# Attention stage of an attention and mixture-of-experts kernel: x kept in SBUF and stored late, k and v products by 128 tokens, two score buffers, normalization on GpSimd

## What is computed

```python
# attention over a memory of 32 slots, for 8 batches x 8 heads, 576 tokens, 64 dims
a = exp(phi - max(phi, tokens)); a = a / (sum(a, tokens) + 1e-9)       # [b h s m]
k_m, v_m = einsum('bhsm,bhsd->bhmd', a, k), einsum('bhsm,bhsd->bhmd', a, v)
scores = q @ k_m.T / sqrt(64); scores -= max(scores, m)
attn = exp(scores); attn = attn / (sum(attn, m) + 1e-9)
x = (attn @ v_m)                       # heads joined: x is [4608 tokens, 512]
# feed-forward, 512 -> 2048 -> 512
h = x @ w_in; x2 = (h * sigmoid(1.702 * h)) @ w_out
# 8 experts, 512 -> 1024 -> 512, each token by the one of its largest logit
e = argmax(x2 @ w_gate); gate = softmax(x2 @ w_gate)[e] * sigmoid(x2 @ w_output_gate)[e]
out = gate * (relu(x2 @ w1[e]) @ w2[e])
```

## Time and profile before

| | |
|---|---|
| device time, median of 3 runs | 1362.95 us (1360.7 to 1366.06) |
| the profiled execution: its own time | 1360.2 us |
| its span, first to last instruction | 1358.1 us |
| mean granted TensorE clock | 0.998 |
| TensorE busy | 1321.8 us, 97% |
| VectorE, ScalarE, GpSimd busy | 660.8, 388.8, 527.6 us |
| HBM read, written | 146.03 MB, 100.45 MB |

### The profile page before, as it was taken

The page is one execution under the profiler, slowest core; times in us unless marked ns, Lnnn a source line. Parts: engine busy times, 40 slices in busy tenths (PEclk is TensorE's granted clock), DMA queues, the critical chain, the costliest instruction groups (busy, mean ns, idle before and its releaser), DMA issues.

```text
span 1358.1 us, 25712 instructions
## 1 busy us (share of the span) xinstructions
PE 1321.8 (97%) x7778; PEld 1075.4 (79%) x7779; DVE 660.8 (49%) x1349; ACT 388.8 (29%) x721; POOL 527.6 (39%) x622
## 2 busy tenths in 40 slices
PE   6888999999999999999999999999999999999997
PEld 4566788888888888888888888887788888888886
DVE  5997243453433433434334344347655555555553
ACT  3554222232222222322223222223322222222221
POOL 2005774453344433433434435511433342433331
PEclk9999999999999999999999999999999999999999
DMA  8996447656565465454654646547873779649882
GB/s 322 391 409 251 139 153 206 201 193 184 189 193 182 160 192 188 169 186 155 185 193 159 184 175 192 176 148 258 238 226 96 219 227 266 169 125 250 259 238 62
DMA packets 155641, 275.28 MB, mean 203 GB/s; under 512 B 17107, under 2 KB 54244, under 8 KB 153540
## 3 DMA queue, kind: packets, MB, share of 16 engines
q1 hardware_dynamic: 98804, 205.35, 44.0%
q10 hardware_dynamic: 43600, 37.37, 11.2%
q0 software_dynamic: 13184, 31.88, 7.5%
HBM read 146.03 MB, written 100.45 MB: 181 GB/s over the span
## 4 chain that ended last, share of the span: by engine, by line
PE 93%; DMA 2%; POOL 1%; ACT 1%; issue 1%; DVE 0%; ACTq 0%; SPq 0%; POOLq 0%; DVEq 0%
PE ps L674 28%; PE ps L707 28%; PE ps L748 16%; PE ps L777 15%; PE ps L633 2%; PE ps L620 1%; PE ps L648 1%; PE ps L717 1%; DMA x2x<-xT_scratch 1%; DMA raw<-in_moe_w_out 1%; PE ps L605 1%; DMA kvm<-in_kv 1%; DMA xT_scratch<-xo 1%; POOL W L1509 0%; POOL xs L1538 0%
## 5 line engine op out<-in xcount | busy, mean ns | idle before, releaser
L674 PE MATMUL ps<-xs,W 128*128 (+1 forms) x1728 | 417.8, 391 | 3.1 <-POOL W L1519 1.6
L707 PE MATMUL ps<-W,gs 128*128 128x512 f32 x1728 | 415.0, 389 | 0.1
L674 PEld LDWEIGHTS ps<-xs,W 128*128 128x128 f32 x1728 | 322.8, 188 | 73.0 <-issue 4.4
L707 PEld LDWEIGHTS ps<-W,gs 128*128 128x128 f32 x1728 | 324.2, 188 | 67.9 <-DVE gs L1205 0.5
L1203 DVE TENSOR_TENSOR gate<-ps,gate 128x512 f32<-128x512 f32 x144 | 99.6, 691 | 358.8 <-ACT gate L931 358.4
L931 ACT ACTIVATE gate<-ps 128x512 f32<-128x512 f32 x144 | 86.1, 598 | 466.3 <-PE ps L674 465.8
L748 PE MATMUL ps<-W,cx 128*128 (+1 forms) x936 | 218.5, 389 | 0.8 <-issue 0.8
L777 PE MATMUL ps<-W,chT 128*128 (+1 forms) x936 | 218.3, 389 | 0.9 <-DVE chT L1340 0.9
L1546 POOL CAST whi<-raw 128x512 fp32r<-128x512 f32 x128 | 85.4, 667 | 319.0 <-DMA raw<-in_moe_w 318.9
L777 PEld LDWEIGHTS ps<-W,chT 128*128 128x128 f32 x936 | 175.5, 188 | 38.1 <-issue 1.7
L748 PEld LDWEIGHTS ps<-W,cx 128*128 128x128 f32 x936 | 175.5, 188 | 37.6 <-issue 1.4
(11 more groups left out here) (158 smaller groups left out, 810.4 us busy)
## 6 DMA issues: line engine op xcount, KB each, us to landing
W<-expert_scratch SPq DMA_DIRECT2D x24, 2048.0 KB, 11.0
raw<-in_moe_w SPq DMA_DIRECT2D x128, 256.0 KB, 2.8
expert_scratch<-whi SPq DMA_DIRECT2D x128, 256.0 KB, 2.6
expert_scratch<-raw SPq DMA_DIRECT2D x128, 256.0 KB, 2.9
cq<-ch ACTq DMA_DIRECT2D x156, 128.0 KB, 3.8
kvm<-in_kv SPq DMA_DIRECT2D x16, 1152.0 KB, 7.1
crec<-record_scratch POOLq DMA_DIRECT2D x160, 64.0 KB, 3.7
qT<-in_q SPq DMA_DIRECT2D x16, 576.0 KB, 6.3
```

What stands on the lines that cost most here:

```text
L674: mm = pe.matmul(ps[:, f % 2, :], W[:, col:col + P], xs[:, bass.ds(x0 + (x_lo * K1 + c) * T, T)], start=(c == 0 and w_lo + x_lo == 0), sto ...
L707: mm = pe.matmul(ps[:, 2 + s, :], gs[:, f % 2, g_lo, s * P:(s + 1) * P], W[:, col:col + DM], start=(f == 0 and g_lo + w_lo == 0), stop=(f ...
```

## The change

- **x kept.** `x_out` copies the attention output of batches 0 to 6 into a buffer `keep` that lies where w_out's half of W comes to lie, and of batch 7 into `xo`. Nothing of x is stored during the groups. ScalarE stores batches 0 to 5 in two DMAs within group 15, batch 6 in two more behind it (`store_kept`), batch 7 in one (`store_last`). GpSimd's split of the first chunk into the `keep` region beyond the first four (f == 4) waits for the stores; SyncE's `load_x(1)` waits for the first of them.
- **Tile 0 of x** is split out of `keep` and isn't loaded: high parts by ScalarE (`first_x_hi`, in group 15), low parts by GpSimd (`first_x_lo`, three) and VectorE (one).
- **k and v products by 128 tokens.** CA = 4 chunks of 128 tokens, and 64 tokens left over: 16 + 4 products instead of 36, four 128x128 transposes and two small ones instead of 18. The host lays out kv and phi to match, in rows of the same length.
- **Next a transposed early.** `exp_phi(g+1)` and the transposes of a for g+1 move into group g, ahead of the k transpose and the scores of g.
- **Two score buffers** `sc[u]`. VectorE's order becomes `phi_in(g+1)`, `inverses(g)` (sums and inverses for the scores of g-2 and, in one more column, for phi of g), `less_max(g-1)`, `attn_out(g-2)`.
- **GpSimd** does the normalizing multiply (`normalize(g-2)`, after `inverses(g)`) and the v blocks (`v_blocks(g)`, from SBUF, scaled by `kv_scale(g)` on ScalarE, which scales k and v in one instruction).
- **Layout of w_in** and of the x rows by 128-row blocks instead of every fourth row; early weight chunks are loaded behind groups 1, 2, 11 and 12.

```diff
-CA = 9
-PA = S // CA
+CA = S // P
+PA = S - CA * P
...
+        KEEP = SLOT // 2
+        KEPT = B - 1
...
-                if not isinstance(g, int) or g >= 4:
-                    store_group(g, b, u)
...
-                if isinstance(g, int) and g < K1 - 1:
-                    load_w(g, w_in_part(g, 0))
-                if isinstance(g, int) and g == NG - 5:
-                    load_w(K1 - 1, w_in_part(K1 - 1, 0))
+                if isinstance(g, int) and 1 <= g < 3:
+                    load_w(g - 1, w_in_part(g - 1, 0))
+                if isinstance(g, int) and g >= NG - 5 and g < NG - 3:
+                    load_w(g - (NG - 5) + 2, w_in_part(g - (NG - 5) + 2, 0))
...
                         if k == 1:
+                            sp.wait_ge(s_xfirst, 16 * 2)
+                            sp.wait_ge(s_pT, NG)
                             load_x(t + 1)
...
+            def a_transposes(g):
+                wait(pe, s_aT, g + 1)
+                for c in range(CA):
+                    pe.transpose(ps[:, 0, c * P:(c + 1) * P], aT[:, c * P:(c + 1) * P], ident[:])
+                for hh in range(2):
+                    rows = slice(hh * PA, (hh + 1) * PA)
+                    tr = pe.matmul(ps[rows, 1, 0:PA], aT[rows, CA * P:S], ident[rows, rows],
+                                   start=True, stop=True, tile_position=(hh * PA, hh * PA))
+                tr.then_inc(s_atr, 1)
             def group(g, b, r):
                 u = r % 2
                 has_out = not isinstance(g, int) or g >= 2
-                wait(pe, s_aT, g + 1)
+                last = isinstance(g, int) and g == NG - 1
+                wait(pe, s_kvl[u], 16 * (b + 1))
+                if not isinstance(g, int) or g >= 3:
+                    wait(pe, s_xo, 2 * g - 5)
+                hold(pe, s_am, g + 1)
+                out_of = lambda h: ps[h * M:(h + 1) * M, 4, 3 * P:4 * P].rearrange("p (w d) -> p w d", w=2)
+                for c in range(CA):
+                    for h in range(HG):
+                        pe.matmul(out_of(h), am[:, c * P + h * M:c * P + (h + 1) * M], kv_main[u][:, :, h, c, :],
+                                  start=(c == 0), stop=False, tile_position=(0, h * M))
+                for h in range(HG):
+                    hh, h2 = h // 2, h % 2
+                    rows = slice(hh * PA, (hh + 1) * PA)
+                    mm = pe.matmul(out_of(h), am[rows, CA * P + h2 * M:CA * P + (h2 + 1) * M], kv_left[u][rows, :, h2, :],
+                                   start=False, stop=True, tile_position=(hh * PA, h * M))
+                mm.then_inc(s_kv, 1)
+                if not last:
+                    a_transposes(g + 1)
                 wait(pe, s_kmT, g)
-                hold(pe, s_vbd, g)
-                for c in range(CA):
-                    for hh in range(2):
-                        rows = slice(hh * PA, (hh + 1) * PA)
-                        tr = pe.matmul(ps[rows, c // 8, (c % 8) * 2 * M:(c % 8 + 1) * 2 * M], aT[rows, c * PA:(c + 1) * PA],
-                                       ident[rows, rows], start=True, stop=True, tile_position=(hh * PA, hh * PA))
-                tr.then_inc(s_atr, 1)
+                hold(pe, s_kk, g + 1)
+                for i in range(2):
+                    tr = pe.matmul(ps[i * D:(i + 1) * D, 1, 3 * P:4 * P], kvs[:, 0:D], ident[:],
+                                   start=True, stop=True, tile_position=(0, i * D))
+                tr.then_inc(s_ktr, 1)
...
+                if has_out:
+                    out_half(g - 2, (r + 2) % 4, 1)
...
+            def store_kept(b, n, stored):
+                act.wait_ge(s_xo, 4 * (b + n))
+                for u in range(2):
+                    act.dma_start(xT_dram[2 * u * P:(2 * u + 2) * P, b * S:(b + n) * S].rearrange("(a p) n -> p a n", a=2),
+                                  keep_v[:, :, kept_at(b, u):kept_at(b + n, u)]).then_inc(stored, 16)
+            def store_last():
...
+            def first_x_hi(c):
+                act.wait_ge(s_sc, NG - 1)
+                act.wait_ge(s_xo, 4)
+                act.copy(xs[:, c * T:(c + 1) * T], kept(c)).then_inc(b_xhi, 1)
             def group(g, b, r):
                 u = r % 2
                 last = isinstance(g, int) and g == NG - 1
-                a_out(g)
-                if not isinstance(g, int) or g:
-                    exp_scores(g - 1)
                 if not last:
                     exp_phi(g + 1, 1 - u)
+                if not isinstance(g, int) or g >= 3:
+                    x_out(g - 3, b - 2 + u, 1 - u, 1)
+                if last:
+                    for c in range(K1):
+                        first_x_hi(c)
+                kv_scale(g, u)
+                if not isinstance(g, int) or g:
+                    exp_scores(g - 1, 1 - u)
+                k_out(g)
+                if not last:
+                    a_out(g + 1)
+                else:
+                    store_kept(0, KEPT - 1, s_xfirst)
                 if not isinstance(g, int) or g >= 2:
                     x_out(g - 2, b - 1, u, 0)
-                k_twice(g, u)
-                k_out(g)
-                if not isinstance(g, int) or g >= 2:
-                    x_out(g - 2, b - 1, u, 1)
...
+            def inverses(g, u, scores, phi):
+                lo, hi = (0 if scores else SB), (SB + 1 if phi else SB)
+                if scores:
+                    wait(dve, s_ex, g - 1)
+                    dve.tensor_reduce(scs[:, u, 1, 0:SB], by_m(u), AX.X, ALU.add).then_inc(s_sm, 1)
+                    wait(dve, s_sm, g - 1)
+                if phi:
+                    wait(dve, s_aT, g + 1)
+                dve.tensor_scalar(scs[:, u, 1, lo:hi], scs[:, u, 1, lo:hi], 1e-9, None, ALU.add).then_inc(s_eps, 1)
+                wait(dve, s_eps, g + 1)
+                dve.reciprocal(scs[:, u, 2, lo:hi], scs[:, u, 1, lo:hi]).then_inc(s_rin, 1)
+            def attn_out(g, u):
+                wait(dve, s_nrm, g + 1)
                 wait(dve, s_o, 2 * g)
-                dve.transpose(pT[:], sc[:]).then_inc(s_pT, 1)
...
+                u = r % 2
                 last = isinstance(g, int) and g == NG - 1
-                if soft:
-                    less_max(g - 1)
+                two = not isinstance(g, int) or g >= 2
                 if not last:
-                    phi_in(g + 1, b + r % 2, 1 - r % 2)
-                k_inverse(g, r % 2)
-                if soft:
-                    inverse(g - 1)
-                    attn(g - 1)
-                v_block(g, r, r % 2)
-                if soft:
-                    attn_out(g - 1)
+                    phi_in(g + 1, b + u, 1 - u)
+                inverses(g, u, two, True)
+                if not isinstance(g, int) or g:
+                    less_max(g - 1, 1 - u)
+                if two:
+                    attn_out(g - 2, u)
...
+            def normalize(g, u):
+                pool.wait_ge(s_rin, g + 3)
+                by_m = sc[u][:].rearrange("p (n m) -> p n m", m=M)
+                pool.tensor_tensor(by_m, by_m, scs[:, u, 2:3, 0:SB].rearrange("p o n -> p n o").broadcast_to([P, SB, M]),
+                                   ALU.mult).then_inc(s_nrm, 1)
+            def v_blocks(g, r):
+                pool.wait_ge(s_kk, g + 1)
+                if g >= 4:
+                    pool.wait_ge(s_o, 2 * (g - 4) + 2)
+                pool.tensor_tensor(vbd[:, r, :].rearrange("p (n d) -> p n d", n=2),
+                                   kvs[:, D:2 * D].rearrange("p (o d) -> p o d", o=1).broadcast_to([P, 2, D]),
+                                   mask[:].rearrange("p (n d) -> p n d", n=2), ALU.mult).then_inc(s_vbd, 1)
+            def first_x_lo(c):
                 pool.wait_ge(b_xhi, c + 1)
-                pool.tensor_tensor(lo, xraw[:, c, :], hi.bitcast(F32), ALU.subtract).then_inc(b_xlo, 1)
+                pool.tensor_tensor(xs[:, (K1 + c) * T:(K1 + c + 1) * T], kept(c), xs[:, c * T:(c + 1) * T].bitcast(F32),
+                                   ALU.subtract).then_inc(b_xlo, 1)
+            pool.wait_ge(s_cst, 2 * 16)
+            for g in range(NG):
+                if g >= 2:
+                    normalize(g - 2, g % 2)
+                if g == NG - 1:
+                    for c in range(2):
+                        first_x_lo(c)
+                v_blocks(g, g % 4)
+                for c, at in enumerate((2, 3, NG - 4, NG - 3)):
+                    if g == at:
+                        split_w_in(c, c, 0)
+            first_x_lo(2)
+            normalize(NG - 2, 0)
+            pool.wait_ge(s_x3, 1)
+            pool.wait_ge(b_xlo, K1 - 1)
+            pool.sem_inc(b_xlo, 1)
...
+                            if f == 4:
+                                kept_stored(pool)
+                            split_w(K1 + 2 * f, 0, f)
```

More of the change, by code:

```diff
@@ L469, in _ @@
                 sp_group(g, g // 2, g % 4)
-            for i in range(2):
-                sp.wait_ge(s_xst[i], 16)
-            load_x(0)
-            for g in range(NG - 4, NG - 2):
```

(5 more changed lines are left out.)

217 lines of the change are left out of this document (95 added, 122 removed).

## The result

The change made the kernel slower: 1370.22 us (median of 4 runs, 1368.63 to 1370.68) against 1361.83 us for the kernel before on the same chip (1359.34 to 1366.06). The ratio is 1.0059, with a 95% interval of 1.0034 to 1.0084. I had predicted 1351. The profiled execution took 1368.63 us, with a span of 1367.0; before it was 1360.2 and 1358.1.

The account below looks back on a forecast made before the run. TensorE, back to back from product mm1(0,4), bounds the kernel, so only that start moves: 95.8+34.5 = 130.3 instead of 142.92, 12.6 less. 1363.0 - 12.6 = 1350.4, with 0.6 back 1351 us; range 1341 to 1363.

Parts of the forecast that it names:

- The loop through SyncE's queue: Attention groups: phi maximum, scores, q and phi issue, phi landing; two groups per round, (7.2+λ)/2, taken as 5.5 us a group.
- λ: Time from issue to landing of a group's phi load: forecast 3.55 us, bounds 2.6 and 7.3.
- pitch: Time from one attention group to the next: forecast 5.5 us instead of 6.64.
- The first groups: Start of the attention stage: group 3's score transposes forecast at 35.3 us instead of 37.5.
- The change-over: From the last groups to the first token tile: weights start at L+7.4, stores slow three chunks, mm1(0,4) starts at L+34.5.
- L: Start of the score transposes of group 14, the second last: forecast 95.8 us instead of 110.52.
- distance: Time from L to the start of product mm1(0,4): forecast 34.5 us, 32.4 before the change.
- the price of the stores: Change-over: late x stores make a weight chunk cost 5.0 us instead of 2.5, for some three chunks.
- the phi loop keeps a late landing: Rival, groups: phi still lands late; slower from L = 108.4, pitch 6.65, λ 6.1; at pitch 7.65, 1374 us; chance 0.12.
- the rival of the starving weights: Rival, change-over: stores starve weights longer or SyncE's wait decides; mm1(0,4) or its equivalent at L+45, 1361 us; chance 0.15.
- signs of being wrong: Phi landing above 6 us, loads staying at 350 GB/s, or the stores outlasting L+30.
- reads are the limit: Rival, groups: loads alone limited to 358 GB/s; pitch 5.8 us, L = 99.1, 1354 us; chance 0.2.
- All hidden: Rival: λ under 3, weight loads undisturbed; pitch 5.15 us, L = 92, 20 us less, 1343 us; chance 0.15.

Follow-up runs that it names:

- e4: The changed kernel with half of each kv load left out from group 2 on: 1365.63 us, ratio 1.0021.
- e3: The changed kernel with the six-batch store cut into eight DMAs with 2,304-byte rows instead of 13,824: 1367.41 us, ratio 1.0028.
- e12: The changed kernel with phi ahead of kv and q, early splits at groups 4, 5, 9, 10, six-batch store issued before ScalarE's group 15 work: 1346.92 us.
- e13: The changed kernel with only the four early weight-chunk splits moved, to groups 4, 5, 9 and 10: 1370.35 us, ratio 1.0054.
- e10: e7 with GpSimd's four early weight-chunk splits moved to groups 4, 5, 9 and 10: 1347.94 us, ratio 0.9892.
- e7: The changed kernel with phi loaded ahead of kv and q, and the late store in 2,304-byte rows: 1355.53 us, ratio 0.9941.
- e11: The changed kernel with phi ahead of kv and q, x stored group by group, early splits at groups 4, 5, 9, 10: 1351.04 us, ratio 0.9919.
- e9: The changed kernel with the two k transposes of each group issued four times to keep TensorE busy: 1369.48 us, ratio 1.005.

## Why the prediction was wrong

**What bounds the kernel:** right. Nothing but the start of mm1(0,4) mattered, apart from 1.7 us near the start of stage C, which I had not looked for and whose cause stays open; no experiment was made on it.

**The loop through SyncE's queue:** the mechanism was right, the size wrong. This is the step that failed first. From the start of the phi maximum to the phi load two groups on, I had 1.9 + 4.7 + 0.6 = 7.2; the trace gives 7.9 on the mean, of which the scores (1.21 us against 0.72) and output halves (1.33 against 0.75) at half clock and the weight loads in SyncE's queue are the visible part. For the landing λ I had 3.55 between 2.6 and 7.3; it is 5.0. Half of (7.9 + 5.0) is 6.45, and the measured pitch 6.43. The 3.55 took phi as standing behind a q load half done and nothing else, with a fixed part of 1.75. The trace shows what that left out: of the eleven phi loads from 32 to 96 us, ten were issued 0.6 to 4.0 us before the kv load ahead of them had landed, and took 4.0 to 7.5 us; the one issued just as kv landed, at 65.80, took 3.5. With half of kv (e4) the two issued after kv had landed took 3.6 and 3.8. So the price was right for a phi behind q alone, as far as three loads show, and what failed is the premise that kv would be through by then. Eleven pitches of 0.93 too little are 10.2 us. At a pitch near the old one every us of λ counts half a us per group, 5.5 over the stage; I had that in my formula and should have seen that the whole gain hung on it.

**The first groups:** group 3 came at 38.8, not 35.3: 3.5 us. Group 0 is 1.7 late, at 19.27 and not 17.6, as phi(2), issued at 5.92, took 12.4 us to land. The next three phi loads landed in 4.1 to 5.6 us, about as the walk had it; the other 1.8 us lie in the way round to their issue, up to 8.7 us, with TensorE at its half level from 28.7 to 35.5 us.

**The change-over:** GpSimd started the weights at L + 7.9, where I had 7.4. The distance was 39.1, and I had 34.5 with bounds of 28 and 35.5: 4.6 us too little, and outside the bounds. I let each engine take turns row by row, which gives 5.0 us a chunk; the first two took 10.7 and 12.7. Shorter rows did bring them to 7.9 and 7.5 (e3), so their length has a part in it; but by turns between rows of nearly equal length a chunk would have been hardly late at all. The Trainium skill (DMA: Bandwidth & Descriptors, Queues, rings and completion order) says that an engine turns between queues a packet of several descriptors at a time. By that rule, applied to the weight rows alone, I had 32.5, further off than my own; I had not asked what it makes of several of the store's rows in one turn, which would hold a chunk longer. No run settles that rule. The runs show only that such a chunk lands when the store ahead of it is nearly through (e12); how an engine shares its time between two queues stays open. This is the second step that failed: the price of the stores, three chunks of 5.0 us.

**Together:** 3.5 + 10.2 + 4.6 = 18.3 us, which is 148.6 against 130.3. With 1.4 for the half clock and 1.7 in stage C, and less the 0.6 that I had put back, it is 20.8; the miss by the spans is 20.9 (8.9 slower where I had 12.0 faster). By the medians the miss is 19.2.

**What I costed at nothing:** the collision of GpSimd and VectorE cost nothing, as forecast; the multiply took 1.16, less than the 1.43. The early splits in GpSimd's queue I had not costed as a wait ahead of the normalization at all. In the kernel as changed that omission is harmless (e13); with the loop gone it is worth 7 us (e10 against e7).

**The rivals:** the nearest is "the phi loop keeps a late landing", with 0.12. It named L = 108.4 as the point from which the kernel is slower; L was 109.5. But it got there by a landing of 6.1 and a pitch of 6.65, where 5.0 and 6.43 were measured, and 3.5 us of that L come from the first groups. With my distance of 34.5 that L alone would have cost 1 us; the rest of the loss is what the rival of the starving weights describes, in part: 39.1, between my 34.5 and its 45. Against the late landing I had held that DMA would idle a third of the time and have no backlog; at a pitch of 6.43 it was busy 0.93, and kv was the backlog. Of my signs of being wrong, phi did not land above 6, but the loads ran at 333 GB/s and the last store landed at 141.1, L + 31.6. The low rate was no limit, and "reads are the limit" was false: 420 GB/s of loads alone in e10, with nothing stored in that window. The Trainium skill gives 358 GB/s as a core's limit (DMA: Bandwidth & Descriptors, Specifications), but the Trainium skill's HBM Reference (Specifications (TRN2)) calls this the share of a core when both of a pair stream, and puts a core alone near 425. This case, on one core, agrees with the latter; I had cited only the former. "All hidden" was not absurd: with phi in front and the splits moved L is 92.0 to 93.0, near its L of 92.

**What the change was worth without these flaws:** 1346.9 to 1347.9, 14 to 15 us faster than before, more than my forecast, with phi in front, the splits moved, and the big store in short rows (e10) or issued earlier (e12). No run has the first two alone. The change freed what I had said it would free; the order of three loads in one queue gave 12 us of it away. Keeping x is the smaller part: with x stored at once (e11) it is 1351.0, 3 to 4 us more, as L comes 12 to 13 us later and the distance is 7 to 10 us shorter.

## What to carry to other kernels

When work moves and a resource is freed, go around the loop that the in-order queues close: which load stands behind which wait, and how long until its use. The load that is used first must not stand behind a wait for something late, even if that wait was free before. An engine that gets time-critical work must not have, ahead of it in the same queue, an operation that waits for a load; that was harmless while the engine had nothing else. And moving stores out of a full stage pays less, or nothing, where they later stand ahead of a load that is waited for, or where the engine that issues them lacks the time.

## What was not expected of the hardware

- A 256 KB load issued behind 7 MB of stores on another queue landed after 9.1 (e12) to 14.0 us (e9), instead of 2.7; with the stores' rows cut from 13,824 to 2,304 bytes it was still 6.8 (e10) to 7.9 us (e3).
- The same 288 KB load of phi landed in 3.5 us when the kv load ahead of it landed just as it was issued, and in 4.0 to 7.5 us when kv was still on its way (the kernel as changed, 32 to 103 us).
- The issue itself can be the cost: two DMAs of 3456 KB in 13,824-byte rows held ScalarE's queue for 0.98 us, eight of 864 KB in 2,304-byte rows for 10.0 us.
- The 16 DMA engines moved 420 GB/s of loads alone (e10, share 1.02), against 358 from 20 to 30 us of the kernel before at 0.96 and 346 at 0.98 after. The busy share did not tell these apart.
- In the kernel as changed TensorE's granted clock fell to its half level in eight stretches between 28.7 and 148.1 us, one of them at 100.3, behind 2.07 us in which TensorE had waited for pT. Having it full from 35 to 97 us (e9) gained 0.7 us, which is no more than the runs scatter.
